# Regrouping the tokens of an attention-to-FFN chain: groups of 2, 4, 4 and 2 units in place of three of 4

## The reference

```
for t in range(S):                       # per batch and head
    m_new = max(f[t] + m, i[t]);  f_s = exp(f[t] + m - m_new);  i_s = exp(i[t] - m_new)
    C = f_s * C + i_s * outer(v[t], k[t]);   n = f_s * n + i_s * k[t]
    y[t] = sigmoid(o[t]) * (C @ q[t]) / max(|n . q[t]|, 1)
x = y as (1536, 320)
h = x @ w_in;  x = (h * sigmoid(1.702 * h)) @ w_out
p = probs / (sum(probs) + 1e-9)
out = sum over e of p[:, e] * (relu(x @ w1[e]) @ w2[e])
```

## Time and profile before

| | |
|---|---|
| median of 3 runs | 660.87 us (659.26 to 663.09) |
| profiled execution | 662.75 us, of which the span (first to last instruction) is 660.2 us |
| PE busy | 613.8 us, 93% of the span |
| PE weight loads | 550.3 us, 83% |
| DVE, ACT, POOL busy | 271.7, 169.3 and 184.3 us |
| chain that ended last | PE 62%, issue 18%, POOL 10%, DVE 5%, ACT 2%, DMA 2% |
| mean granted clock of PE | 0.995 |

### The profile page before, as it was taken

The page is one execution under the profiler, slowest core; times in us unless marked ns, Lnnn a source line. Parts: engine busy times, 40 slices in busy tenths (PEclk is TensorE's granted clock), DMA queues, the critical chain, the costliest instruction groups (busy, mean ns, idle before and its releaser), DMA issues.

```text
span 660.2 us, 9849 instructions
## 1 busy us (share of the span) xinstructions
PE 613.8 (93%) x3748; PEld 550.3 (83%) x3748; DVE 271.7 (41%) x521; ACT 169.3 (26%) x360; POOL 184.3 (28%) x117
## 2 busy tenths in 40 slices
PE   3765899999999999879999999999999999999998
PEld 2764688897888887769899899999978899998898
DVE  2334354454554556654533333333323333333333
ACT  2443453334433333221211111111111111111120
POOL 3566553341633413664302232032220000000000
PEclk9999999999999999998999999999999999999999
DMA  5973233211330001223010111001110000000012
GB/s 183 298 256 92 93 94 93 80 58 48 92 91 1 0 0 49 88 88 128 0 49 1 41 49 40 24 26 40 49 42 1 1 0 1 1 1 0 1 41 79
DMA packets 11603, 38.25 MB, mean 58 GB/s; under 512 B 1552, under 2 KB 3504, under 8 KB 11568
## 3 DMA queue, kind: packets, MB, share of 16 engines
q1 hardware_dynamic: 11568, 37.75, 17.6%
HBM read 35.68 MB, written 2.06 MB: 57 GB/s over the span
## 4 chain that ended last, share of the span: by engine, by line
PE 62%; issue 18%; POOL 10%; DVE 5%; ACT 2%; DMA 2%; SPq 1%; POOLq 0%; ACTq 0%; DVEq 0%
PE bank L400 10%; PE bank L402 10%; PE bank L401 10%; PE bank L392 7%; PE bank L393 7%; PE bank L391 7%; POOL g_lo L216 4%; PE bank L388 4%; PE bank L389 4%; DVE g_lo L216 2%; POOL qc L783 2%; POOL dn_lo L770 1%; DMA qk<-qk_d 1%; DVE gbuf L665 1%; ACT gbuf L544 1%
## 5 line engine op out<-in xcount | busy, mean ns | idle before, releaser
L400 PE MATMUL bank<-dn_hi,g_lo 128*128 128x320 f32 x576 | 181.8, 316 | 7.7 <-DVE ysum L673 6.3
L402 PE MATMUL bank<-dn_hi,g_hi 128*128 128x320 f32 x576 | 179.0, 311 | 0.0
L401 PE MATMUL bank<-dn_lo,g_hi 128*128 128x320 f32 x576 | 178.7, 310 | 0.0
L587 ACT ACTIVATE g_hi<-bank 128x512 fp32r<-128x512 f32 x96 | 57.4, 598 | 274.1 <-PE bank L393 274.1
L400 PEld LDWEIGHTS bank<-dn_hi,g_lo 128*128 128x128 f32 x576 | 108.8, 189 | 11.1 <-DVE ysum L673 7.1
L749 DVE SCALAR_TENSOR_TENSOR g_lo<-bank,g_hi 128x512 fp32r<-128x512 f32 x96 | 66.3, 692 | 120.5 <-ACT g_hi L587 120.2
L391 PE MATMUL bank<-xT,up_hi 128*128 128x512 f32 (+1 forms) x288 | 113.1, 393 | 0.0
L392 PE MATMUL bank<-xT,up_lo 128*128 128x512 f32 (+1 forms) x288 | 113.1, 393 | 0.0
L393 PE MATMUL bank<-xT,up_hi 128*128 128x512 f32 (+1 forms) x288 | 112.8, 392 | 0.0
L401 PEld LDWEIGHTS bank<-dn_lo,g_hi 128*128 128x128 f32 x576 | 109.0, 189 | 1.1
L402 PEld LDWEIGHTS bank<-dn_hi,g_hi 128*128 128x128 f32 x576 | 108.9, 189 | 0.0
(11 more groups left out here) (99 smaller groups left out, 558.2 us busy)
## 6 DMA issues: line engine op xcount, KB each, us to landing
up_raw<-up_d SPq DMA_DIRECT2D x12, 768.0 KB, 5.4
dn_raw<-down_d SPq DMA_DIRECT2D x12, 640.0 KB, 4.0
negB<-floors_d SPq DMA_DIRECT2D x12, 512.0 KB, 3.8
kvo<-kvo_d SPq DMA_DIRECT2D x12, 488.0 KB, 5.6
qk<-qk_d SPq DMA_DIRECT2D x24, 160.0 KB
carB<-carries_d SPq DMA_DIRECT2D x24, 80.0 KB
out_d<-acc SPq DMA_DIRECT2D x2, 640.0 KB, 3.3
out_d<-acc SPq DMA_DIRECT2D x4, 160.0 KB, 1.8
```

What stands on the lines that cost most here:

```text
L400: mm(dst[:, 0:DM], g_lo[:, par, f, toks], dn_hi[s][:, f, :], start=f == 0, stop=False)
L401: mm(dst[:, 0:DM], g_hi[:, par, f, toks], dn_lo[s][:, f, :], start=False, stop=False)
L402: last = mm(dst[:, 0:DM], g_hi[:, par, f, toks], dn_hi[s][:, f, :], start=False, stop=f == NF - 1)
L587: go(g_hi[:, j % 2, f, :], UPB[f][:, :], ACT.Relu).then_inc(hi2_done, 1)
```

## The change

The FFN's token groups become 2, 4, 4 and 2 units (`GROUPS`), written out one after the other, without a loop. Only units 0 and 1 run alone, in an order written out by hand. Group 0 (units 0 and 1) has units 2 to 5 beside it, one every 5 slots; group 1 (units 2 to 5) has units 6 to 9 beside it, one every 7; group 2 (units 6 to 9) has units 10 and 11 beside it, one every 12; group 3 (units 10 and 11) runs without attention. A group of two units has 24 slots, with up tiles of 256 columns.

Only block 0 of the weights is split in the time alone. Of blocks 1 to 3 each part is split in a slot of group 0 (`SPLIT_SLOTS`): ACT makes the high part after that slot's own work and before its attention stages, and then DVE the low part of an up block, POOL that of a down block. `gbuf` has four places in place of two. In the last group up tiles go round four PSUM banks. `keep_warm` is gone; the last result of a group is transposed after the first up tile of the next, into the `NUM` banks. SP's loads of the weights are interleaved anew with those of units 1 to 3.

```diff
+GROUPS = ((0, 2), (2, 4), (6, 4), (10, 2))
+LAST = len(GROUPS) - 1
-BESIDE_PITCH = 7
+PITCH = (5, 7, 12)
+SPLIT_SLOTS = {0: ("up", 1), 2: ("down", 1), 5: ("up", 2), 8: ("down", 2), 11: ("up", 3), 14: ("down", 3)}
+def moe_slots(gi):
+    count = GROUPS[gi][1]
+    slots = [("up", 0, f) for f in range(NF)]
+    for q in range(1, HB1):
+        slots += [("up", q, f) for f in range(NF)] + [("down", q - 1, k) for k in range(count)]
+    return slots + [("down", HB1 - 1, k) for k in range(count)]
+def att_stages(gi, slot):
+    if gi == LAST:
+        return []
+    first, count = GROUPS[gi + 1]
+    return [(first + q, stage) for q in range(count) for stage in BESIDE if slot == PITCH[gi] * q + BESIDE[stage]]
...
-    gbuf, _, _ = sb("gbuf", [P, 2, FB], F32)
+    gbuf, _, _ = sb("gbuf", [P, NF, FB], F32)
+    def up_free(gi, q, i):
+        return up_tile_no(gi, q, i) - (3 if gi == LAST else 1)
+    def up_bank(gi, i):
+        return UPB[i] if gi == LAST else UPB[i % 2]
...
 # SP
+        def load_unit(u):
+            if u > 1:
+                sp.wait_ge(y_done, u - 1)
+            load_rows(u, u % 2)
+            load_qk(u, u % 2)
+            load_kvo(u, u % 2)
+        load_unit(1)
+        load_up(0)
+        load_down(0)
+        load_up(1)
+        load_unit(2)
+        load_down(1)
+        load_up(2)
+        load_unit(3)
+        load_down(2)
+        load_up(3)
+        load_down(3)
...
 # PE, units alone
+        attention(0, -1, SCORE)
+        attention(0, -1, INTER)
+        attention(0, -1, STATE)
+        attention(1, -1, SCORE)
+        attention(0, -1, VALUES)
+        attention(1, -1, INTER)
+        attention(1, -1, STATE)
+        attention(0, -1, TRANSPOSE)
+        attention(1, -1, VALUES)
+        attention(1, -1, TRANSPOSE)
...
 # PE, a group
-            pe.wait_ge(num_read, units)
-            keep_warm(NUM[1], 6)
-            out_transpose(g, UPG - 1, units)
-            pe.wait_ge(x2lo_done, UPG * g + UPG)
+                    up_tile(up_bank(gi, i), q, i, toks).then_inc(up_done, 1)
+                    if slot == 0 and gi > 0:
+                        out_transpose(first - 1, gi - 1)
...
 # ACT, a slot: tanh, then the pending g_hi, then
+                if gi == 0 and slot in SPLIT_SLOTS:
+                    weights_hi(*SPLIT_SLOTS[slot])
+                for u, stage in att_stages(gi, slot):
+                    attention(u, gi, stage)
 # ACT, units alone
+        attention(0, -1, EXPS)
+        attention(0, -1, GATE)
+        attention(1, -1, EXPS)
+        weights_hi("up", 0)
+        weights_hi("down", 0)
+        attention(0, -1, TRANSPOSE)
...
 # DVE, a slot: gbuf or ysum, then
+                if gi == LAST and slot > 0 and slots[slot - 1][0] == "up":
+                    lo1(dve, v, gi, *slots[slot - 1][1:])
+                if gi == 0 and slot in SPLIT_SLOTS and SPLIT_SLOTS[slot][0] == "up":
+                    up_split(SPLIT_SLOTS[slot][1])
 # DVE, units alone
+        attention(0, -1, WEIGH)
+        attention(0, -1, STATE)
+        attention(1, -1, WEIGH)
+        up_split(0)
+        attention(0, -1, FINISH)
...
 # POOL, a slot of groups 0 to 2: attention, lo1, then
+                if gi == 0 and slot in SPLIT_SLOTS and SPLIT_SLOTS[slot][0] == "down":
+                    down_split(SPLIT_SLOTS[slot][1])
```

More of the change, by code:

```diff
@@ L72, with up_tile_no, down_tile_no @@
 EARLY = (WEIGH,)
-BESIDE_PITCH = 7
[L74 to L86, removed]
+PITCH = (5, 7, 12)
[6 more added lines that the diff above has]
+    return slots + [("down", HB1 - 1, k) for k in range(count)]
+def up_tile_no(gi, q, i):
+    return NF * (HB1 * gi + q) + i
+def down_tile_no(gi, q, k):
+    first, count = GROUPS[gi]
+    return HB1 * first + count * q + k
+def att_stages(gi, slot):
[3 more added lines that the diff above has]
+    return [(first + q, stage) for q in range(count) for stage in BESIDE if slot == PITCH[gi] * q + BESIDE[stage]]
 def build(nc, gates_d, ident_d, probs_d, qk_d, kvo_d, up_d, down_d, floors_d, carries_d, out_d):
@@ L403, in down_tile, with out_transpose @@
             return last
-        def ffn_group(g, with_attention):
-            units = UPG * (g + 2) if with_attention else NU
-            for slot, (kind, q, i) in enumerate(MOE_SLOTS):
-                n = HB1 * g + q
+        def out_transpose(v, gi):
+            first, count = GROUPS[gi]
+            pe.wait_ge(dn_read, down_tile_no(gi, HB1 - 1, v - first) + 1)
+            pe.wait_ge(num_read, min(first + count + GROUPS[min(gi + 1, LAST)][1], NU))
+            if v >= 2:
+                pe.wait_ge(x2lo_done, v)
+            transposes(NUM[v % 2], ysum[:, v - first, :]).then_inc(x2T_done, 1)
@@ L430, in ffn_group @@
[L430 to L442 removed]
+                        out_transpose(first + i - 1, gi)
@@ L540, in ffn_group @@
+        def ffn_group(gi):
+            first, count = GROUPS[gi]
+            width = count * P
+            pending = None
+            for slot, (kind, q, i) in enumerate(moe_slots(gi)):
+                tile = up_tile_no(gi, q, i)
                 if kind == "up":
                     act.wait_ge(up_done, tile + 1)
-                    if slot >= 2:
-                        act.wait_ge(glo_done, tile - 1)
-                    go(gbuf[:, i % 2, :], UPB[i % 2][:, :], ACT.Tanh, scale=GELU / 2).then_inc(tanh_done, 1)
+                    if tile >= NF:
+                        act.wait_ge(glo_done, tile - NF + 1)
+                    go(gbuf[:, i, 0:width], up_bank(gi, i)[:, 0:width], ACT.Tanh, scale=GELU / 2).then_inc(tanh_done, 1)
@@ L566, in _ @@
-        act.wait_ge(ident_in, 16)
-        go(ident_b[:, :], ident[:, :], ACT.Copy)
+                    pending = (q, i)
+                if gi == 0 and slot in SPLIT_SLOTS:
+                    weights_hi(*SPLIT_SLOTS[slot])
+                for u, stage in att_stages(gi, slot):
+                    attention(u, gi, stage)
+                if slot == 0 and gi > 0:
+                    out_hi(first - 1)
+                if kind == "down" and q == HB1 - 1 and i >= 1:
+                    out_hi(first + i - 1)
```

337 lines of the change are left out of this document (144 added, 193 removed).

## The result

The changed kernel takes 662.96 us (median of 20 runs, 660.17 to 665.75), the kernel before 660.52 us (20 runs, 658.69 to 663.09). The ratio is 1.0039 with a 95% interval of 1.0025 to 1.0052: 2.4 us slower. That is less than the 0.5% that the prediction called no change, but the interval lies above 1: a small loss, and no gain. Forecast was a gain of 4.8 us to 656.1. The measured time lies in the range of 646 to 667.

A forecast was written before the change was run, and what follows sets the result against it. PE bounds full groups and the second FFN, but not the units alone or the last group. 42.0 + 76.8 + 82.3 + 70.5 + 35.0 + 0.5 + 348.3 = 655.4 us span against 660.2; median forecast 656.1, range 646 to 667.

The forecast's parts named there:

- the clock behind the stalls: Group 0: half clock after each of three stalls costs about 1.65 us, 5.0 in all.
- the lock in the last group: Last group: g_lo on DVE beside POOL's splits makes PE lose 3.0 us, plus 1.0 for the clock; group 35.0.
- one execution for another: Profiled execution before took 662.75 us, median 660.87; a gain of 4.8 was applied to the median, giving 656.1.
- The first up tile: End of the units alone: the first up tile starts at 42 us (40 to 46), 26.9 earlier.
- The width: Two-unit groups: 256-column matmuls at 0.120 us each make up tiles cost 1.6 us more than one four-unit group's.
- The three stalls: Group 0, slots 7, 12 and 17: SCORE waits behind ACT's queue for 6, 5.9 and 4.0 us, together 15.9.
- The loads: Weight loads queued behind unit 3's land at 50 to 57 us, before ACT wants them at about 65 and 75: hidden.
- Groups 1 and 2: Middle groups: 82.3 us for group 1 and 70.5 for group 2, without new waits.
- Rival 1: Group 0 stalls only by the bare 1.7 us each: group 0 at 61, time 640; chance 0.12.
- Rival 2: Group 0: splits on POOL or DVE hold the recurrence, SCORE stalls reach 9 us; group 88, time 667; chance 0.2.
- Rival 3: Last group: every g_lo meets a split, another 6.3 us, time 662; chance 0.15.
- Rival 4: Units alone: unit 1's data land as late as before, 4.7 us later, time 661; chance 0.08.

The follow-up runs named there:

- Experiment 1: Changed kernel with 59 idle 512-column matmuls in group 0's four PE waits, before TRANSPOSE of unit 2 and SCORE of units 3 to 5: 651.09 us.
- experiment 7: Changed kernel with POOL's splits of blocks 5 to 7 held until every g_lo of the last group is done: 654.99 us.
- experiment 4: Changed kernel with group 0's weight splits moved to slots 0, 3, 4, 8, 9 and 13: 660.35 us.
- experiments 2 and 3: Changed kernel, group 0 only: EXPS one slot later, 656.48 us; separately, TRANSPOSE at offset 6 in place of 7, 653.64 us.
- experiment 9: Changed kernel with TRANSPOSE at offset 6, splits moved, POOL's blocks 5 to 7 held, and 20 idle matmuls before unit 2's TRANSPOSE: 644.16 us.
- experiment 6: Changed kernel with TRANSPOSE at offset 6, splits moved, and 6, 6, 8, 6 idle matmuls before unit 2's TRANSPOSE and units 3 to 5's SCORE: 655.87 us.
- experiment 12: Kernel of experiment 10 with 12, 6 and 14 idle matmuls ahead of the TRANSPOSE of units 2, 3 and 4: 650.98 us.
- experiment 10: Changed kernel with TRANSPOSE at offset 6, no weight split in slots 1 to 6 of group 0, and POOL's blocks 5 to 7 held: 646.26 us.

## Why the prediction was wrong, step by step

**The failed step: the clock behind the stalls.** "Three such stalls cost about 1.65 each, 5.0." They cost about 10.5. Group 0 after has 64.29 us of busy PE and 15.49 of idle PE. The prediction had 53.1 + 1.6 + 5.0 = 59.7 busy and 1.2 + 15.9 = 17.1 idle. So the idle time was 1.6 too dear and the busy time 4.6 too cheap, which is the +3.0 of the stage. Experiment 1 measures the term. There the clock was held and the waits were filled with 13.4 us of idle matmuls (59 x 0.227), with 1.2 us of idle time left: about as long as the waits before. The rest of PE's busy time is 67.7 - 13.4 = 54.3, which is 10.0 less than the 64.3 of the kernel after. The start of the stage has to be set apart, as the prediction did. Both kernels begin the stage at half speed, with 256-column matmuls 0.214 apart, until 44.5 after and 45.5 in experiment 1 (the column of the granted clock reads 1.00 there and does not show it; the second pair of rows is at full speed); by the difference to 0.120 that is some 1.3 and 1.9 us lost, for 1.6 forecast. It leaves 54.3 - 1.9 = 52.4 for the work at full clock, for 53.1 forecast, and 64.3 - 52.4 - 1.3 = 10.6 behind the stalls, twice the 5.0. These are estimates from the rows.

```profile
43.85 0.41 PE L405 MATMUL bank<-xT,up_hi 128*128 128x256 f32 x1
44.06 0.41 PE L406 MATMUL bank<-xT,up_lo 128*128 128x256 f32 x1
...
45.12 0.28 PE L405 MATMUL bank<-xT,up_hi 128*128 128x256 f32 x1
45.24 0.28 PE L406 MATMUL bank<-xT,up_lo 128*128 128x256 f32 x1
```

The price had been read from a stall in the last group, behind which half clock lasted 3.4 us with large matmuls following; behind the stalls of group 0 it lasted 4.5, 9.4 and about 10 us. Behind the two long ones SCORE, INTER and small up tiles follow; behind the short one SCORE and then a down tile of twelve 320-column matmuls.

**The second failed step: the lock in the last group.** Predicted were 30.5 of PE, 0.5 for a read, 3.0 for the wait and 1.0 for the clock. Undisturbed the group takes 32.86 (experiment 7: 30.85 busy, 2.0 idle, of which 1.47 is PE's wait for the last `xT`, a term left out). Of the 5.7 us above that, PE idled 3.9 for the lock, and was busy for 1.8 more by the clock. The mechanism and the place were right, the sum too small by 3.6, of which the left-out wait is 1.5. In experiment 4's profile, with a wait of 5.73, the group took 41.5, near the upper end of the stated 31 to 42.

**The third: one execution for another.** The profile of before was taken as the measure of the kernel, and 1.9 us was given off to its median. The median of after lies 2.0 above its own profile, and it ran 0.8 less outside the span than before's 2.55. So the miss of 6.9 us (662.96 less 656.1) is 3.8 in the stages, 2.0 and 1.9 in the draws, less 0.8. The draws go with the clock: of the 20 runs after, those at a mean granted clock of 0.977 had spans of 658.4 and 659.2, the five at 0.969 had 661.2 to 663.9. Between 0.977 and 0.969 lie some 10 us of half clock (0.008 x 659 x 2), which cost up to 5, an estimate. Part of the 2.0 is likely the last group's wait, which in the profiled execution was shorter than in the others named above; no run separates the two.

**What held.** The first up tile at 41.55 for 42.0. The width: 256-column matmuls start 0.1195 us apart for 0.120. The three stalls, their place and their sum, and with experiments 2 and 3 a large part of their cause: what stands ahead of `split_hi` on ACT. ACT's rows ahead of slot 12's SCORE are the list that the prediction gave, the high part of `up3` included:

```profile
77.20 1.48 ACT L582 ACTIVATE up_hi<-up_raw 128x1536 fp32r<-128x1536 f32 x1
78.58 2.43 ACT L532 ACTIVATE pT<-negB,aT 128x128 f32<-128x128 f32 x8
80.92 0.36 ACT L561 ACTIVATE gbuf<-bank 128x256 f32<-128x256 f32 x1
81.18 0.41 ACT L565 ACTIVATE g_hi<-gbuf 128x256 fp32r<-128x256 f32 x1
81.48 0.37 ACT L520 ACTIVATE xT<-bank 128x256 fp32r<-128x256 f32 x1
```

The split by stall was less good: slot 7 has 3.37 in front of SCORE and 3.53 in front of TRANSPOSE (6 forecast), slot 12 4.89 (5.9), slot 17 3.20 (4.0). The loads stayed hidden. Groups 1 and 2 were 1.3 and 0.9 shorter than forecast, with PE busy for nearly all of it.

**The rivals.** Rival 1 did not occur. Rival 2's mechanism did, in its first instance only: STATE's step took 2.75 us in place of 0.33.

```profile
51.40 2.93 POOL L804 TENSOR_TENSOR dn_lo<-dn_raw,dn_hi 128x1280 fp32r<-128x1280 f32 x1
...
51.77 2.75 DVE L636 TENSOR_TENSOR state<-state,decay 128x168 f32<-128x168 f32 x1
```

With the 2.23 us of `up_lo` that stood ahead of FINISH, it made the 3.53 in front of unit 2's TRANSPOSE. The next link is there too: POOL's scaled queries (`qc`) took 2.78 us beside that `up_lo`, 1.30 elsewhere, so ACT got its exponents late and EXPS of unit 3 began at 59.63, ahead of the `split_hi` for which SCORE waited. But the two waits of that slot came to 6.9 us, no slot reached 9, and group 0 stayed under the 81.6 from which that rival decides. The rule of the Trainium skill (SBUF — State Buffer, "SBUF: two separate sides"), that a DVE operation with two SBUF inputs and a GpSimd operation that reads SBUF shut each other out for a whole instruction, agrees with these rows: the DVE step, begun inside POOL's, ended 0.19 us after it. Rival 3 is half true: not every `g_lo` met a split, but PE lost 3.9 us and not 3.0. Rival 4 did not occur.

**What stays open.** Why some executions of one kernel have longer half clock than others, and what sets its length behind a stall. That the small matmuls make it long is argued from where they stand; no run put large ones in their place and left the stall. They are not all of it: in the last group, where the same 320-column matmuls follow the same wait, half clock lasted 3.4 us behind 3.95 us of waiting (the kernel after) and nearly 6 behind 4.11 (experiment 1).

## What to carry to other kernels

A wait in a stretch of small matmuls can cost more in the clock behind it than in itself: price it by rows from a stretch of the same kind, and take the longest as the bound. Idle matmuls in a wait hold the clock, but whether they pay must be measured: they took 11.9 us off in experiment 1 and brought group 0 nothing in experiment 9. In experiments 6 and 12 they made group 0 2.1 us longer and 2.8 shorter, and both kernels came out 5 us slower, mostly in the second FFN, where PE paused for a reason that stays open. A stage that looks bound by PE's tiles may be bound by DVE and POOL locking each other out: starting POOL's splits some us later was worth 7 to 8 us in both groupings, about as much as the regrouping, which gained nothing as written and 5 to 7.5 us rearranged. Take the time before from several executions, since the one that was profiled can lie 0.3% off.

## What the runs showed of the hardware

**Half clock outlasts the stall by very different times.** Behind 3.33 us idle with large matmuls following, 3.4 us. Behind 4.11 us with the same kind following, nearly 6 (experiment 1's last group):

```profile
292.13:298.13 6.00, 6.00 (x23) 6.00 (x24) 0.79 (x2) 0.00 (x0) 5.88 (x3) 0.50 0.16 65
```

Behind 4.89 and 3.20 us with attention's small ones among those that follow, 9.4 and about 10, but behind 3.53 and 3.37 close together 4.5. Behind only 2.27 us, 12 us or more (experiment 10).

**PE pauses when the second FFN's loop starts its second pass**, half way through that stage, and in experiments 6 and 9 once more 4 to 5 us later, with "issue" in place of a releaser. It took 0.98 to 1.54 us in eleven of the fourteen kernels profiled, 1.24 and 1.67 in experiment 9, 0.97 and 3.72 in experiment 6 and 5.63 in experiment 12, and the clock was at 0.50 for 3.9 us behind the last. The three kernels with long pauses are three of the four that have idle matmuls added; experiment 1 has the most of them (59) and paused 1.28. So the number of instructions alone does not set it. Near the pause one packet of a DMA queue named "instruction" is seen in experiments 6, 9 and 12, but also in experiment 10, whose pause is one of the short ones (0.98), so the packet alone does not tell them apart. The cause is not settled.
